# Splitting the first expert's weights during the recurrence instead of during the routing

## The chip, the cores and the metric

One Trainium2 chip, one core. The time is the device time in microseconds of one launch of the whole program; the number that counts is the median of several runs. TensorE is called PE, VectorE DVE, ScalarE ACT, GpSimd POOL, and SyncE, which issues most DMAs, SP.

## The reference

Three layers on N = 10112 tokens (2 sequences of 5056) of width 256. First a gated recurrence, then two mixture-of-experts layers with 8 experts each and one expert per token:

```
f = lower_bound + (1 - lower_bound) * sigmoid(f_logit);  i = 1 - f
h_t = f_t * h_(t-1) + i_t * x_t                      # over the sequence
# MoE (twice; the first with normalized rows and embeddings and a temperature)
e = argmax(logits);  g = softmax(logits)[e]
out = g * (relu(h @ w1[e]) @ w2[e])                  # w1: 256 x 1024, w2: 1024 x 256, fp32
```

## The kernel before

The program has one instruction stream per engine, tied together by semaphores that are written out by hand. Three stages follow one another.

**Recurrence.** The 79 tiles of 128 tokens are taken in 20 chunks (`NCH`) of 4 tiles. For chunk k, PE transposes x and f_logit (`a_front`, L1203), in two halves of 128 features; ACT takes the tanh `th` of the gate half (L1049), POOL turns it into the gate `fg` (L888), DVE makes the product `gx` (L371) and the scan `hT` (L381). A chunk later `a_back` follows: PE transposes `hT` back (L1216) and multiplies it for the router logits (L1222), ACT copies the rows to `h_rows` (L1059) and takes the eight squares and sums `sq` (L1063), which signals `rows_ok`; DVE copies the logits (`keep_logits`, L389), which signals `lg_kept`. PE's next `a_back` waits for `rows_ok` and, ahead of the logits, for `lg_kept`. On SP, step k issues the loads of chunk k + 4 (`load_chunk`, L737; they wait until the transposes of chunk k are done), and then the store of chunk k (`store_chunk`, L745; it waits for `rows_ok`). Each load or store is 512 KB (1.57 MB a chunk). All engines go through steps 0, 1, 2, ... in order; the first steps are unrolled and the rest are in a loop.

**Routing.** DVE finds the largest logit, counts tokens per expert and builds a table of slots with one-hot products on PE (L1240). `slot_row` (L485) tells which row of the scratch tensor `rows_a` goes to which slot. POOL copies two columns of it for each pair of tiles (`places`, L950) and gathers the rows with indirect DMAs (`gather`, L966). PE waits for DVE's mark "table read", and then for the gathered rows (L1290).

**Experts.** 94 steps (47 pairs of tiles per layer), each with the weights of one expert. All products are in fp32r in three parts: a weight matrix is split into a high part, which ACT copies from `w1raw` to `w1h` (`split_w1_hi`, L1032) or from `w2raw` to `w2h` (`split_w2_hi`, L1040), and a low part, the difference, which DVE writes to `w1l` (`split_w1_lo`, L355) or `w2l` (`split_w2_lo`, L362). Each split is two instructions of 128 x 1024. In the steps, the weights of the next expert are loaded and split beside the matmuls of this one (L1306 for the first product, L1324 for the second). For the first pair (`Index(0)`, always expert 0) this has to be done ahead of the steps: SP issues the two loads of 1 MB (L759, L767) behind the store of the last chunk, ACT splits the high parts at the start of its routing, and DVE the low parts between `slot_row` and the mark "table read":

```
link(v.scalar_tensor_tensor(slot_row[:, :], v0, float(P), v1, ALU.mult, ALU.add))
mark["slots"] = count[0]
for c in range(DC):
    split_w1_lo(Index(0), c)
for half in range(2):
    split_w2_lo(Index(0), half)
link(v.tensor_scalar(empty[:, :], v1, 0.0, None, ALU.is_equal))
mark["table read"] = count[0]
```

The constant `SPLIT_K` is 3 and is used nowhere in this kernel but in an assertion.

Of the kernel before, what the change touches and what calls it, by code (L numbers as in the profile page):

```python
# [31 lines left out]
def wait(eng, sem, value):  # L32

    if isinstance(value, int) and value <= 0:
        return
    eng.wait_ge(sem, value)
# [16 lines left out]
def build(nc, x, f_logit, lower_bound, emb, tau, w1a, w2a, w_gate, w1b, w2b, out):  # L53
# [9 lines left out]
    DC = D // P  # L63
# [8 lines left out]
    NCH = -(-TT // CH)  # L72
# [12 lines left out]
    def tiles_in(k):  # L85
        return min(CH, TT - k * CH)
# [10 lines left out]
    with ctx:  # L97
# [178 lines left out]
        def layer_of(i):  # L276
            return loop_layer[0] if i.var is not None else i.const // NP

        def par(i):
            return i.const % 2  # L280

        def pair_uses(i, slots=2, scale=16):
            return i.uses(slots, scale)
# [27 lines left out]
        SPLIT_K = 3  # L311
# [6 lines left out]
        def _(dve):  # L318
            count = [0]

            def link(ins):

                ins.then_inc(dve_c, 1)
                count[0] += 1
                dve.wait_ge(dve_c, count[0])
# [25 lines left out]
            def split_w1_lo(i, c):  # L351

                cols = slice(c * F, (c + 1) * F)
                wait(dve, w1_hi, i.value(2, c + 1))
                v.tensor_tensor(w1l[:, par(i), cols], w1raw[:, par(i), cols],  # L355
                                w1h[:, par(i), cols].bitcast(fp32), ALU.subtract).then_inc(w1_lo, 1)

            def split_w2_lo(i, half):

                cols = slice(half * (WE // 2), (half + 1) * (WE // 2))  # L360
                wait(dve, w2_hi, i.value(2, half + 1))
                v.tensor_tensor(w2l[:, par(i), cols], w2raw[:, par(i), cols],  # L362
                                w2h[:, par(i), cols].bitcast(fp32), ALU.subtract).then_inc(w2_lo, 1)


            def a_step(i, nt=CH, edge=None):
                w = nt * P
                par = i.const % 2
                for c in range(DC):
                    wait(dve, f_ok, i.value(2, c + 1))  # L370
                    v.scalar_tensor_tensor(gx[:, c, 0:w], fg[:, c, 0:w], 1.0, bank[c][:, 0:w],  # L371
                                           ALU.subtract, ALU.mult).then_inc(g_ok, 1)
                    wait(dve, g_ok, i.value(2, c + 1))
                    if edge is not None:

                        link(v.memset(fg[:, c, edge:edge + 1], 0.0))

                    wait(dve, lg_ok, i.value(1, -1))
                    wait(dve, rows_ok, i.value(1, -1))
                    wait(dve, h_ok, i.value(2, c - 1))  # L380
                    v.tensor_tensor_scan(hT[:, c, par, 0:w], fg[:, c, 0:w], gx[:, c, 0:w],  # L381
                                         hT[:, c, 1 - par, CW - 1:CW], ALU.mult,
                                         ALU.subtract).then_inc(h_ok, 1)
                if i.var is not None or i.const > 0:
                    keep_logits(i.plus(-1), CH)

            def keep_logits(k, nt):
                wait(dve, lg_ok, k.value(1, 1))
                v.tensor_copy(logit[:, bass.ds(k.value(CH), nt), :],  # L389
                              bank[6][:, 0:nt * E].rearrange("p (t e) -> p t e", e=E)  # L390
                              ).then_inc(lg_kept, 1)
# [10 lines left out]
            def routing():  # L402
# [81 lines left out]

                link(v.scalar_tensor_tensor(slot_row[:, :], v0, float(P), v1, ALU.mult, ALU.add))  # L485
                mark["slots"] = count[0]
                for c in range(DC):
                    split_w1_lo(Index(0), c)
                for half in range(2):
                    split_w2_lo(Index(0), half)  # L490
                link(v.tensor_scalar(empty[:, :], v1, 0.0, None, ALU.is_equal))
                mark["table read"] = count[0]

# [230 lines left out]
        def _(sp):  # L724
# [6 lines left out]
            def load_chunk(k, nt):  # L731

                slot_x = k.const % XS
                wait(sp, turned, k.value(2, 2 - 2 * XS))
                k0 = k.value(CH)
                for dst, src in ((xin, x_v), (fin, f_v)):
                    sp.dma_start(dst[:, slot_x, 0:nt * D].rearrange("p (t d) -> p t d", d=D),  # L737
                                 src[:, bass.ds(k0, nt), :]).then_inc(xf_in[slot_x], 16)

            def store_chunk(k, nt):  # L740

                par = k.const % 2
                wait(sp, rows_ok, k.value(1, 1))
                k0 = k.value(CH)
                sp.dma_start(rows_av[:, bass.ds(k0, nt), 0:D],  # L745
                             h_rows[:, par, 0:nt * D].rearrange("p (t d) -> p t d", d=D)
                             ).then_inc(h_out[par], 16)
# [3 lines left out]
            def first_expert(i):  # L751
                return i.var is None and i.const == 0

            def load_w1(i):

                w1 = weights[layer_of(i)][0]
                wait(sp, w1_lo, i.value(2, -2))
                src = w1[0:1, :, :] if first_expert(i) else w1[bass.ds(expert_of(i), 1), :, :]
                sp.dma_start(w1raw[:, par(i), :].rearrange("p (c f) -> p c f", c=DC),  # L759
                             src.rearrange("o (c p) f -> p (o c) f", p=P)).then_inc(w1_in[par(i)], 16)  # L760

            def load_w2(i):

                w2 = weights[layer_of(i)][1]
                wait(sp, w2_lo, i.value(2, -2))
                src = w2[0:1, :, :] if first_expert(i) else w2[bass.ds(expert_of(i), 1), :, :]
                sp.dma_start(w2raw[:, par(i), :].rearrange("p (c d) -> p c d", c=FC),  # L767
                             src.rearrange("o (c p) d -> p (o c) d", p=P)).then_inc(w2_in[par(i)], 16)
# [6 lines left out]
            def expert_of(i):  # L775
                return sp.snap(expert_reg[par(i)], min_val=0, max_val=E - 1)
# [9 lines left out]
            def a_step(i):  # L786
                whole = i.var is not None
                if whole or i.const + XS < NCH:
                    load_chunk(i.plus(XS), CH if whole else tiles_in(i.const + XS))
                store_chunk(i, CH if whole else tiles_in(i.const))  # L790
                if i.var is None and i.const == NCH - 1:
                    load_w1(Index(0))
                    load_w2(Index(0))

            run_steps(sp, 0, NCH, a_step, LOOP_K - 3, 5)

            def store_y(i):
# [222 lines left out]
        def _(act):  # L1020
# [6 lines left out]
            def split_w1_hi(i, c):  # L1027

                cols = slice(c * F, (c + 1) * F)
                wait(act, w1_in[par(i)], pair_uses(i) + 16)  # L1030
                wait(act, up_ok, i.value(JS, -JS))
                nc.scalar.activation(w1h[:, par(i), cols], w1raw[:, par(i), cols],  # L1032
                                     ACT.Copy).then_inc(w1_hi, 1)

            def split_w2_hi(i, half):

                cols = slice(half * (WE // 2), (half + 1) * (WE // 2))
                wait(act, w2_in[par(i)], pair_uses(i) + 16)
                wait(act, down_ok, i.value(JS, -JS))
                nc.scalar.activation(w2h[:, par(i), cols], w2raw[:, par(i), cols],  # L1040
                                     ACT.Copy).then_inc(w2_hi, 1)


            def a_front(k, nt):
                w = nt * P
                for c in range(DC):
                    wait(act, turned, k.value(2, c + 1))
                    wait(act, f_ok, k.value(2, c - 1))
                    nc.scalar.activation(th[:, c, 0:w], bank[2 + c][:, 0:w], ACT.Tanh,  # L1049
                                         scale=0.5).then_inc(tanh_ok, 1)  # L1050
# [15 lines left out]

            def a_step(i):
                a_front(i, CH if i.var is not None else tiles_in(i.const))
                if i.var is not None or i.const > 0:
                    a_back(i.plus(-1), CH)  # L1070

# [9 lines left out]

            def routing():

                for c in range(DC):
                    split_w1_hi(Index(0), c)
                for half in range(2):
                    split_w2_hi(Index(0), half)
                act.wait_ge(lg_ok, NCH)
                act.wait_ge(shift_ok, 2)
                nc.scalar.activation(ex[:, 0:TT, :], shifted[:, 0:TT, :], ACT.Exp).then_inc(act_s, 1)  # L1090
                for q, t0 in enumerate(range(0, TT, RC)):
                    scaled(q, min(RC, TT - t0), ST)
# [317 lines left out]
```

## Time and profile before

| | |
|---|---|
| median of 3 runs | 1382.35 us (1382.05 to 1383.36) |
| profiled execution: time / span | 1383.36 / 1381.6 us |
| busy: PE / DVE / ACT / POOL | 96% / 70% / 60% / 32% of the span |
| recurrence | to about 112 us |
| routing | about 112 to 169 us |
| experts | 169 us to the end |
| bytes moved | 276.83 MB, mean 200 GB/s |

A row of the timeline gives start, duration, engine (PEld is the weight load of PE, SPq the issue of a DMA on SP), line, operation, output and inputs, the count of instructions merged into it, and in brackets the idle time of the engine ahead of it with what ended it. Times in it count from the start of the span. "x2 ... 2.36" is two instructions that together took 2.36 us.

### The profile page before, as it was taken

The page shows a single profiled execution, that of the slowest core. Times are in us where ns is not written, and L with a number is a line of the kernel's source. Part 1 is how long each engine was busy: PE and PEld are TensorE (multiplying, and loading weights), DVE is VectorE, ACT ScalarE, POOL GpSimd, SP SyncE. Part 2 cuts the span into 40 slices and gives each one's busy share as a digit, 9 for nine tenths or more (in the row PEclk, how much of TensorE's full clock was granted, in tenths as well). Part 3 has the DMA queues.
Part 4 walks back from the last instruction along what each step waited for, and adds up shares of the span by engine and source line. Part 5 has one row for each costly group of instructions (what it writes and reads, how often), then busy time and mean ns, then how long its engine had stood idle before and what let it go on. Part 6 is the DMA issues. An engine that isn't in the chain of part 4 may idle for free.

```text
span 1381.6 us, 31343 instructions
## 1 busy us (share of the span) xinstructions
PE 1329.6 (96%) x11005; PEld 1299.6 (94%) x11005; DVE 971.5 (70%) x1468; ACT 835.2 (60%) x1402; POOL 439.2 (32%) x458
## 2 busy tenths in 40 slices
PE   7994799999999999999999999999999999999996
PEld 6993399999999999999999999899999999999996
DVE  5878476666666666669876679777777777777773
ACT  4774166666666666666656566556666666666663
POOL 4663221121221211222111234323444444444431
PEclk9995599999999999999999999999999999999999
DMA  8983686666665656668856668546666666666650
GB/s 256 329 275 104 64 273 193 213 199 194 203 198 200 199 195 214 198 193 154 254 166 192 209 202 217 174 153 212 221 217 213 226 226 216 221 213 219 222 186 1
DMA packets 204662, 276.83 MB, mean 200 GB/s; under 512 B 33350, under 2 KB 171988, under 8 KB 204596
## 3 DMA queue, kind: packets, MB, share of 16 engines
q1 hardware_dynamic: 191060, 240.74, 56.7%
q0 software_dynamic: 13536, 35.21, 7.6%
q8 instruction: 41, 0.67, 0.2%
q14 instruction: 25, 0.20, 0.1%
HBM read 242.69 MB, written 35.18 MB: 201 GB/s over the span
## 4 chain that ended last, share of the span: by engine, by line
PE 91%; DVE 4%; issue 1%; ACT 1%; POOL 1%; DMA 1%; SPq 0%; ACTq 0%; DVEq 0%; POOLq 0%
PE bank L1306 39%; PE bank L1324 38%; PE bank L1240 4%; PE bank L1290 3%; PE bank L1335 2%; PE bank L1344 1%; PE bank L1203 1%; PE bank L1222 1%; PE bank L1216 1%; DVE hT L381 1%; DVE gx L371 1%; POOL fg L888 1%; ACT sq L1063 0%; DMA fin<-in_f_logit 0%; ACT th L1049 0%
## 5 line engine op out<-in xcount | busy, mean ns | idle before, releaser
L1306 PE MATMUL bank<-xs,w1h 128*128 128x256 f32 x3008 | 570.5, 288 | 1.5 <-DVE xs L656 1.5
L1119 ACT ACTIVATE hh<-bank 128x512 fp32r<-128x512 f32 x376 | 225.2, 599 | 413.6 <-PE bank L1306 413.6
L1306 PEld LDWEIGHTS bank<-xs,w1h 128*128 128x128 f32 x3008 | 461.5, 189 | 3.2 <-DVE xs L656 1.9
L667 DVE SCALAR_TENSOR_TENSOR hl<-bank,hh 128x512 fp32r<-128x512 f32 x376 | 259.9, 691 | 249.3 <-ACT hh L1119 246.9
L1324 PE MATMUL bank<-w2h,hl 128*128 128x256 f32 x1504 | 423.1, 281 | 0.0
L1324 PE MATMUL bank<-w2l,hh 128*128 128x256 f32 x1504 | 422.5, 281 | 0.0
L1324 PE MATMUL bank<-w2h,hh 128*128 128x256 f32 x1504 | 421.7, 280 | 0.0
L1306 PE MATMUL bank<-xs,w1l 128*128 128x256 f32 x1504 | 421.6, 280 | 0.0
L1306 PEld LDWEIGHTS bank<-xs,w1l 128*128 128x128 f32 x1504 | 283.7, 189 | 0.0
L1324 PEld LDWEIGHTS bank<-w2h,hh 128*128 128x128 f32 x1504 | 283.3, 188 | 0.0
L1324 PEld LDWEIGHTS bank<-w2l,hh 128*128 128x128 f32 x1504 | 283.1, 188 | 0.0
L1324 PEld LDWEIGHTS bank<-w2h,hl 128*128 128x128 f32 x1504 | 283.0, 188 | 0.0
L355 DVE TENSOR_TENSOR w1l<-w1raw,w1h 128x1024 fp32r<-128x1024 f32 x188 | 230.2, 1225 | 45.0 <-ACT w1h L1032 44.8
L362 DVE TENSOR_TENSOR w2l<-w2raw,w2h 128x1024 fp32r<-128x1024 f32 x188 | 230.4, 1226 | 43.1 <-ACT w2h L1040 42.2
L966 POOL DMA_INDIRECT xb<-rows_a,row_i x94 | 110.2, 1172 | 459.1 <-DVE meta L660 440.8
L976 POOL DMA_INDIRECT out_y<-yb,tok x94 | 125.8, 1338 | 313.0 <-DVE tok L675 282.9
L1032 ACT ACTIVATE w1h<-w1raw 128x1024 fp32r<-128x1024 f32 x188 | 197.6, 1052 | 7.1 <-DMA w1raw<-in_moe_w 7.1
L1040 ACT ACTIVATE w2h<-w2raw 128x1024 fp32r<-128x1024 f32 x188 | 197.6, 1052 | 0.8 <-DMA w2raw<-in_moe_w 0.8
L966 POOL DMA_INDIRECT xb<-rows_b,row_i x94 | 107.7, 1146 | 67.0 <-DVE meta L660 29.7
L1135 ACT ACTIVATE yb<-bank,meta 128x256 f32<-128x256 f32 x188 | 78.6, 470 | 11.4 <-PE bank L1324 4.5
L656 DVE TENSOR_TENSOR xs<-bank,xs 128x512 fp32r<-128x512 f32 x94 | 64.9, 690 | 11.5 <-ACT xs L1113 8.9
L1240 PE MATMUL bank<-vals,lane_oh 128*128 128x124 bf16 (+2 forms) x237 | 59.3, 415 | 10.7 <-DVE vals L511 10.5
(160 smaller groups left out, 1039.6 us busy)
## 6 DMA issues: line engine op xcount, KB each, us to landing
w1raw<-in_moe_w SPq DMA_DIRECT2D x94, 1024.0 KB
w2raw<-in_moe_w SPq DMA_DIRECT2D x94, 1024.0 KB, 5.6
rows_b<-yb SPq DMA_DIRECT2D x94, 128.0 KB, 2.3
xin<-in_x SPq DMA_DIRECT2D x19, 512.0 KB, 6.0
fin<-in_f_logit SPq DMA_DIRECT2D x19, 512.0 KB, 7.9
rows_a<-h_rows SPq DMA_DIRECT2D x19, 512.0 KB, 5.6
xb<-rows_a,row_i POOLq DMA_INDIRECT x94, 4.9
xb<-rows_b,row_i POOLq DMA_INDIRECT x94, 4.9
```

The costliest lines, as they stand in the source:

```text
L355: v.tensor_tensor(w1l[:, par(i), cols], w1raw[:, par(i), cols], w1h[:, par(i), cols].bitcast(fp32), ALU.subtract).then_inc(w1_lo, 1)
L362: v.tensor_tensor(w2l[:, par(i), cols], w2raw[:, par(i), cols], w2h[:, par(i), cols].bitcast(fp32), ALU.subtract).then_inc(w2_lo, 1)
L667: v.scalar_tensor_tensor(hl[:, j, :], bank[j % UB][:, :], 0.0, hh[:, j, :].bitcast(fp32), ALU.max, ALU.subtract).then_inc(hid_lo, 1)
L966: pool.indirect_dma_start(xb[:, s, :], None, rows_of(i), bass.IndirectOffsetOnAxis(row_i[:, s:s + 1], 0)).then_inc(x_in[s], 16)
L976: pool.indirect_dma_start(out, bass.IndirectOffsetOnAxis(tok[:, s:s + 1], 0), yb[:, s, :], None, bounds_check=N - 1, oob_is_err=False).the ...
L1032: nc.scalar.activation(w1h[:, par(i), cols], w1raw[:, par(i), cols], ACT.Copy).then_inc(w1_hi, 1)
L1040: nc.scalar.activation(w2h[:, par(i), cols], w2raw[:, par(i), cols], ACT.Copy).then_inc(w2_hi, 1)
L1119: nc.scalar.activation(hh[:, j, :], bank[j % UB][:, :], ACT.Relu).then_inc(hid_hi, 1)
L1135: nc.scalar.activation(yb[:, s, :], bank[Y_BANK + par(i)][:, t * D:(t + 1) * D], ACT.Copy, scale=meta[:, bass.ds(in_layer(i).value(2 * G, ...
L1240: ins = mm(bank[b][:, 0:2 * W], lane_oh[:, g % RS, :, t], vals[:, g % RS, 0:2 * W, t], start=first and t == 0, stop=last and t == w - 1)
L1306: ins = mm(bank[j % UB][:, f * GW:(f + 1) * GW], w[:, p, o:o + P], xs[:, p, a, c * GW:(c + 1) * GW], start=k == 0, stop=k == 3 * DC - 1)
L1324: ins = mm(bank[Y_BANK + p][:, t * D:(t + 1) * D], a[:, j, f * GW + t * P:f * GW + (t + 1) * P], w[:, p, o:o + D], start=(j, t, f, k) == ( ...
```

## The change

The first expert's weights are loaded and split during the recurrence. SP issues the load of w1 in its step 0 and the load of w2 in its step 1, each behind the load and the store of that step. ACT splits the high parts of w1 in its step 3, between `a_front(3)` and `a_back(2)`, and those of w2 in its step 4, between `a_front(4)` and `a_back(3)`. DVE splits the low parts in the same steps, behind the scans and ahead of `keep_logits`. They are taken out of the routing of both engines. The instructions themselves, their number and their data stay the same.

```
--- before.py
+++ after.py
@@ DVE, a_step @@
                     v.tensor_tensor_scan(hT[:, c, par, 0:w], fg[:, c, 0:w], gx[:, c, 0:w],
                                          hT[:, c, 1 - par, CW - 1:CW], ALU.mult,
                                          ALU.subtract).then_inc(h_ok, 1)
+                if i.var is None and i.const == SPLIT_K:
+                    for c in range(DC):
+                        split_w1_lo(Index(0), c)
+                if i.var is None and i.const == SPLIT_K + 1:
+                    for half in range(2):
+                        split_w2_lo(Index(0), half)
                 if i.var is not None or i.const > 0:
                     keep_logits(i.plus(-1), CH)
@@ DVE, routing @@
                 mark["slots"] = count[0]
-                for c in range(DC):
-                    split_w1_lo(Index(0), c)
-                for half in range(2):
-                    split_w2_lo(Index(0), half)
                 link(v.tensor_scalar(empty[:, :], v1, 0.0, None, ALU.is_equal))
@@ SP, a_step @@
                 store_chunk(i, CH if whole else tiles_in(i.const))
-                if i.var is None and i.const == NCH - 1:
+                if i.var is None and i.const == 0:
                     load_w1(Index(0))
+                if i.var is None and i.const == 1:
                     load_w2(Index(0))
@@ ACT, a_step @@
                 a_front(i, CH if i.var is not None else tiles_in(i.const))
+                if i.var is None and i.const == SPLIT_K:
+                    for c in range(DC):
+                        split_w1_hi(Index(0), c)
+                if i.var is None and i.const == SPLIT_K + 1:
+                    for half in range(2):
+                        split_w2_hi(Index(0), half)
                 if i.var is not None or i.const > 0:
                     a_back(i.plus(-1), CH)
@@ ACT, routing @@
-                for c in range(DC):
-                    split_w1_hi(Index(0), c)
-                for half in range(2):
-                    split_w2_hi(Index(0), half)
                 act.wait_ge(lg_ok, NCH)
```

## Rows read from the trace of the kernel before

**Rows 1.** The page: busy time and share of each engine, and the chain by line.

```profile
PE 1329.6 (96%) x11005; PEld 1299.6 (94%) x11005; DVE 971.5 (70%) x1468; ACT 835.2 (60%) x1402; POOL 439.2 (32%) x458
...
PE bank L1306 39%; PE bank L1324 38%; PE bank L1240 4%; PE bank L1290 3%; PE bank L1335 2%; PE bank L1344 1%; PE bank L1203 1%; PE bank L1222 1%; PE bank L1216 1%; DVE hT L381 1%; DVE gx L371 1%; POOL fg L888 1%; ACT sq L1063 0%; DMA fin<-in_f_logit 0%; ACT th L1049 0%
```

**Rows 2.** Busy time by window: start:end, length, each engine's busy time, clock, DMA.

```profile
8.00:20.00 12.00, 10.22 (x48) 9.48 (x48) 6.06 (x7) 3.31 (x6) 5.96 (x4) 1.00 1.04 333
...
34.00:38.00 4.00, 3.88 (x36) 3.64 (x35) 3.44 (x5) 3.04 (x12) 3.01 (x3) 1.00 1.10 303
...
88.00:92.00 4.00, 4.00 (x24) 4.00 (x23) 2.42 (x5) 2.04 (x8) 0.79 (x2) 0.57 1.06 326
```

**Rows 3.** The timeline of the recurrence, steps 2 to 6.

```profile
22.07 0.51 SPq L737 DMA_DIRECT2D xin<-in_x  x1
...
26.84 0.51 SPq L737 DMA_DIRECT2D xin<-in_x  x1
...
28.68 1.09 ACT L1059 ACTIVATE h_rows<-bank 128x512 f32<-128x512 f32 x2 [0.72 <-PE bank L1216]
...
30.98 0.24 ACT L1063 ACTIVATION_READ_ACCUMULATOR sq<-bank 128x1 f32 x1
...
31.30 0.60 ACT L1049 ACTIVATE th<-bank 128x512 f32<-128x512 f32 x1
...
31.93 0.17 DVE L389 COPY logit<-bank 128x32 f32<-128x32 f32 x1
...
32.80 0.69 DVE L371 SCALAR_TENSOR_TENSOR gx<-fg,bank 128x512 f32<-128x512 f32 x1 [0.71 <-POOL fg L888]
...
35.81 0.60 ACT L1049 ACTIVATE th<-bank 128x512 f32<-128x512 f32 x1
...
39.40 0.63 PE L1203 MATMUL bank<-ident,xin 128*128 128x128 f32 x4
```

**Rows 4.** The timeline: the first transposes of chunks 16 and 17.

```profile
87.73 0.83 PE L1203 MATMUL bank<-ident,xin 128*128 128x128 f32 x4
...
93.75 0.64 PE L1203 MATMUL bank<-ident,xin 128*128 128x128 f32 x4
```

**Rows 5.** The loads of L737 issued in 20:24, then those of 24:36.

```profile
DMA to landing us min/median/max: 5.9/6.8/7.7
...
DMA to landing us min/median/max: 5.7/7.0/8.3
```

**Rows 6.** The first expert's loads and high splits in the timeline; landing of L767.

```profile
112.83 0.47 SPq L759 DMA_DIRECT2D w1raw<-in_moe_w  x1
...
119.46 2.00 ACT L1032 ACTIVATE w1h<-w1raw 128x1024 fp32r<-128x1024 f32 x2 [7.09 <-DMA w1raw<-in_moe_w]
...
122.28 2.00 ACT L1040 ACTIVATE w2h<-w2raw 128x1024 fp32r<-128x1024 f32 x2 [0.81 <-DMA w2raw<-in_moe_w]
...
DMA to landing us min/median/max: 8.9/8.9/8.9
```

**Rows 7.** The timeline behind the routing tables.

```profile
158.81 2.36 DVE L355 TENSOR_TENSOR w1l<-w1raw,w1h 128x1024 fp32r<-128x1024 f32 x2
...
159.00 2.21 POOL L950 COPY row_i<-slot_row 128x2 int32<-128x2 int32 x2 [36.81 <-DVE slot_row L485]
...
161.09 2.35 DVE L362 TENSOR_TENSOR w2l<-w2raw,w2h 128x1024 fp32r<-128x1024 f32 x2
...
161.40 2.01 POOL L966 DMA_INDIRECT xb<-rows_a,row_i  x1 [0.18 <-POOL row_i L950]
...
163.71 1.32 POOL L966 DMA_INDIRECT xb<-rows_a,row_i  x1 [0.31 <-issue]
```

**Rows 8.** All copies of L950 and gathers of L966: duration min/median/max in ns.

```profile
L950 POOL COPY row_i<-slot_row x94: 183/202/1187, 159.0 to 1323.3; 128x2 int32 x56, 128x2 int32<-128x2 int32 x38
...
L966 POOL DMA_INDIRECT xb<-rows_a,row_i x94: 942/973/2023, 161.4 to 747.4; - x94
```

**Rows 9.** The chain that ended last: the second gather to its landing.

```profile
163.71 3.11 DMA xb<-rows_a,row_i
```

## The prediction

> **What bounds the kernel now.** I read the page first. TensorE (PE) is busy for 96% of the span and holds nearly all of the chain that ended last, three quarters of it in the two expert products (L1306, L1324) [rows 1]. The change touches none of those matmuls. It can only move the time at which they start, so I asked the trace two questions: what paces the recurrence stage, where work is put in, and what the last step before the first expert matmul waits for, where work is taken out.
>
> The busy time by window answers the first. In 34 to 38 us PE is busy 3.88 of 4.00 us, VectorE (DVE) 3.44, ScalarE (ACT) 3.04, and the DMA share is 1.10 [rows 2]. No engine has room for a long instruction. The timeline shows how they hang together: ACT's first tanh of a chunk starts right behind the eight squares of `a_back` (30.98 + 0.24, then th at 31.30), DVE waits 0.71 us for the gate of that tanh, and the same tanh one chunk on starts at 35.81 [rows 3]. From front(6) at 39.40 to front(16) at 87.73 a chunk takes 48.33 / 10 = 4.83 us [rows 3, 4].
>
> For the second question, in the timeline after the routing tables, behind slot_row, DVE does the four low-part splits from 158.81, 2.36 and 2.35 us for two each, until 163.44. GpSimd (POOL) meanwhile needs 2.21 us for two copies of two columns and 2.01 us for its first gather; the medians of these are 0.202 and 0.973 us each [rows 7, 8]. The copies end at 161.21 and the gather at 163.41, each just as a pair of splits ends. The chain that ended last runs through POOL here: gather at 161.40, second gather issued at 163.71 and landed 3.11 us later, at 166.82, and from there to the first expert matmul [rows 7, 9].
>
> **Part 1, taken out of the routing end.** Four DVE splits (4.6 us) go from between `slots` and `table read`. PE's wait for `table read` isn't what it waits for last; the second gather is. So what counts is how much sooner POOL gets through. With medians: copies from 159.00 to 159.40, gap 0.18, gather to 160.6, gap 0.31, gather to 161.9; from the end of issue to landing it now takes 3.11 − 1.32 = 1.79, so landing at 163.7, that is 3.2 us sooner. Against it, the small DVE operations for `empty` and `experts` now start at 158.8 and fall on POOL's work. The second gather shows the price: 1.32 instead of 0.97 [rows 7, 8]. If each of the four POOL instructions is held by 0.35, 1.4 us are lost, and the gain is 1.8. I take **2.8**, between 1.8 and 3.2, since two of those are very short. The second expert's loads, which wait for `experts`, are issued sooner too, but behind the four POOL instructions, and PE shows no wait for weights on the chain.
>
> The Trainium skill, "SBUF — State Buffer", section "SBUF: two separate sides", says that DVE and GpSimd share one port pair as an exclusive lock, and that a DVE instruction with two SBUF inputs holds it whole against a GpSimd instruction that reads SBUF. The splits have two such inputs, and the trace agrees: POOL's 2.21 and 2.01 us end with them. By the rule only the two-input ones among the small operations could still block, which would put the gain near the upper end.
>
> **Part 2, taken out of the routing start.** ACT's four splits ran from 119.46 to 124.28 while the weights landed [rows 6]. DVE is then busy with the counting that sets the path, and waits for nothing of ACT before the one-hots. This gains 0.
>
> **Part 3, put into the recurrence: ACT.** Step 3 gets `split_w1_hi` twice behind its tanhs and before `a_back(2)`; step 4 gets `split_w2_hi` twice before `a_back(3)`. Two cost 2.00 us [rows 6]. ACT is in order, so `h_rows`, the squares, `rows_ok` (hence SP's store and the next loads), and the next chunk's tanhs wait behind them, and more so if the weights aren't there. W1 is issued where the loads of chunk 5 are now (22.07), W2 about 26.9 [rows 3]. When do they land?
> - Lower bound: the same transfers of before, on an emptier queue: w1 at 112.83, used at 119.46, 6.6 us; w2 8.9 us [rows 6]. That gives w1 at 28.7, w2 at 35.8.
> - Upper bound: W1 (1 MB) replaces the 1 MB of chunk 5, whose second half landed 7.7 us after its issue at 22.6 (22.07 + 0.51), at 30.3. W2 replaces chunk 6's 1 MB, landed 8.3 us after 27.4 (26.84 + 0.51), at 35.7, pushed back by W1: 1.05 MB at the 333 GB/s that the queue gave in 8 to 20 us is 3.1 us [rows 2, 5]. That gives 38.8.
> The queue is full here, so I take **38.0** for W2. ACT's own earliest is about 35, so W1's exact landing no longer matters. Then: splits to 40.0, `a_back(3)` takes 31.22 − 28.68 = 2.54, so the tanh of chunk 5 starts at 42.6 instead of 35.81: **6.8 late** (4.6 with W2 at 35.8, 7.6 at 38.8) [rows 3].
>
> **Part 3, DVE.** The low splits add 2.36 and 2.35 us [rows 7] behind the scans, before `keep_logits`, on which PE's next logits wait. They end near 34.4 instead of 32.1, and the gate product of 32.80 starts about 1.9 late; the second pair repeats it: 3.8 [rows 3, 7]. This runs beside ACT's 6.8 and isn't added; it is the floor. Two small waits in the loop (0.71 of DVE, 0.72 of ACT before h_rows, [rows 3]) close up as everyone is late, so I let 1.0 be recovered: 6.8 − 1.0 = **5.8** (from 3.8, the DVE floor, to 7.6).
>
> **Clock.** PE will stand still for some 2 to 3 us twice (until rows(2), until rows(3)). The trace shows one fall of the granted clock in this stage, 0.57 in 88 to 92 us, where PE had barely paused; that chunk took 93.75 − 87.73 = 6.02, 1.2 over the average [rows 2, 4]. I expect one or two falls, partly inside time that PE waits anyway: **0.6** (0 to 2.4). The skill's "TensorE: Matmul & The Clock Gate", "HAM oscillation — how this bites in real kernels", speaks against the change: idle gaps of PE are paid a second time at half clock. By that each gap would cost a whole 1.2, and the result would be some 2 us worse; the one fall of this trace came without such a gap.
>
> **DMA.** 2.1 MB more at 333 GB/s make the later loads 6.3 us late. Chunk 6's landed at 35.7 for a use at 39.40, slack 3.7 [rows 3, 5]. So they need the stage to be at least 2.6 late, and it is 5.8: no added cost, but a floor of 2.6 under any luckier case.
>
> **Sum.** 5.8 + 0.6 − 2.8 = **+3.6 us**. The profiled execution took 1383.36 for a span of 1381.6, so 1387.0 on its own; it is 1.0 above the median of the three. On the median: 1382.35 + 3.6 = **1386.0**. Bounds: 3.8 + 0 − 3.2 = +0.6, and 7.6 + 2.4 − 1.8 = +8.2. 0.2% is 2.8 us, about what can be told from no change.
>
> **Rivals.**
> - *Same mechanism, smaller.* W2 lands near 35.8 and PE's stalls are partly made good: PE's 3.88 of 4.00 leaves 0.12 in 4 us, over 15 chunks of 4.83 some 2 us. Then 3.8 to 5 − 2.8: about +1.5, 1383.9. For it: W1 alone took only 6.6 us. Against: the full queue. Chance 0.30.
> - *Faster.* The splits are hidden, because each of ACT and DVE waits 0.7 us a chunk and the delay is worked off by the end of the stage; only the routing end counts. It decides from the point where the stage ends under 2.8 late. Full hiding gives −2.8, 1379.6. Against it: PE, at 97%, can't catch up, and the loads alone hold a floor of 2.6. Chance 0.08.
> - *The loads become the bound.* Each later chunk waits for its loads after W1 and W2, with less than 333 GB/s for mixed traffic (303 in 34 to 38, [rows 2]), or the clock falls twice at full price: 8 to 11 − 2.8, +6.5, 1388.9. Chance 0.14.
> - *No effect at either end* (POOL is still held, and the stage absorbs): 0.03.
> The forecast itself holds 0.45.
>
> **Range and chances.** The forecast and the two neighbours: 1381.5 to 1390.5. Slower by over 0.2% takes most of the forecast and all of the third rival: 0.57. Within 0.2%: the rest of the forecast, the first rival, the last, some of the second: 0.36. Faster: 0.07.
>
> **What the profile after would show.** Right: w2h starting near 38 behind an ACT wait for w2raw, the squares of chunk 3 ending near 42.6, PE idle for 2 to 3 us around 34 and 41, the stage's last squares some 5 to 7 us later than now; POOL's two copies under 1 us, the second gather landed within 5.5 us of the first copy's start (159.00 to 166.82, 7.8, now). Wrong: ACT doesn't wait for w2raw (then +1 to +2), the offset of the chunks shrinks steadily towards the end of the stage (hidden), or PE waits for xin or fin (loads bound).

## The result

The changed kernel takes 1391.57 us (median of 4, 1390.43 to 1392.94) against 1382.41 us before: a ratio of 1.0067, 95% interval 1.0055 to 1.0081. It is 9.2 us slower, where +3.6 was predicted. Two later measurements, each beside the kernel before on the same chip, gave 1.0069 (1.0055 to 1.0082) and 1.0071 (1.0057 to 1.0085).

The page after, with the lines that answer to [rows 1] and the granted clock in 40 slices:

```profile
span 1390.7 us, 31342 instructions
...
PE 1333.7 (96%) x11005; PEld 1303.6 (94%) x11005; DVE 971.2 (70%) x1468; ACT 834.7 (60%) x1402; POOL 434.4 (31%) x458
...
PEclk9796589999999999999999999999999999999998
```

The clock's row began 9995599 before; now its second slice, 35 to 70 us, reads 7. PE's busy time has grown by 4.1 us (1333.7 against 1329.6) with the same 11005 matmuls. The timeline of the recurrence, beside [rows 3]:

```profile
26.36 0.66 SPq L769 DMA_DIRECT2D w2raw<-in_moe_w  x1
...
28.57 2.01 ACT L1035 ACTIVATE w1h<-w1raw 128x1024 fp32r<-128x1024 f32 x2 [1.13 <-DMA w1raw<-in_moe_w]
```

```profile
31.37 2.33 DVE L355 TENSOR_TENSOR w1l<-w1raw,w1h 128x1024 fp32r<-128x1024 f32 x2
...
33.15 1.06 PE L1221 MATMUL bank<-ident,hT 128*128 128x128 f32 x8 [1.58 <-ACT sq L1066]
...
37.83 2.00 ACT L1043 ACTIVATE w2h<-w2raw 128x1024 fp32r<-128x1024 f32 x2 [3.86 <-DMA w2raw<-in_moe_w]
...
38.92 2.36 DVE L362 TENSOR_TENSOR w2l<-w2raw,w2h 128x1024 fp32r<-128x1024 f32 x2 [0.62 <-ACT w2h L1043]
...
42.12 1.12 ACT L1052 ACTIVATE th<-bank 128x512 f32<-128x512 f32 x2
...
42.41 1.94 PE L1221 MATMUL bank<-ident,hT 128*128 128x128 f32 x8 [2.59 <-ACT sq L1066]
...
44.14 3.42 PE L1227 MATMUL bank<-en_T,hT 128*128 128x8 f32 x16
...
47.42 1.09 PE L1208 MATMUL bank<-ident,xin 128*128 128x128 f32 x4
```

W1 landed before 28.57 (ACT idle 1.13). W2, issued at 26.36, kept ACT idle for 3.86 us, and its first high split starts at 37.83; the forecast had 38.0. The tanhs of chunk 5 follow at 42.12, against 35.81 in [rows 3], 6.3 late (forecast 6.8). PE stood still for 1.58 and 2.59 us for the rows (L1066), where 2 to 3 us twice were forecast. Up to here the forecast holds. Then the sixteen small matmuls of the logits take 3.42 us at 44.14, where the kernel before needs 1.85:

```profile
42.28 1.85 PE L1222 MATMUL bank<-en_T,hT 128*128 128x8 f32 x16
```

The busy time by window (window, its length, busy time of PE, PEld, DVE, ACT, POOL, granted clock, DMA share, GB/s), to set beside [rows 2]:

```profile
32.00:36.00 4.00, 2.85 (x24) 2.88 (x25) 3.38 (x5) 1.98 (x8) 2.41 (x3) 0.92 1.11 295
36.00:40.00 4.00, 3.82 (x18) 3.42 (x18) 3.35 (x4) 2.17 (x3) 0.09 (x1) 0.50 1.10 350
40.00:44.00 4.00, 1.59 (x8) 1.62 (x9) 1.73 (x4) 3.24 (x12) 1.15 (x2) 0.50 1.10 329
44.00:48.00 4.00, 4.00 (x21) 4.00 (x20) 3.68 (x5) 2.54 (x10) 1.34 (x2) 0.50 1.04 304
48.00:52.00 4.00, 4.00 (x21) 4.00 (x20) 0.78 (x2) 1.19 (x2) 0.77 (x1) 0.50 1.08 292
52.00:56.00 4.00, 4.00 (x37) 3.97 (x36) 3.25 (x4) 3.12 (x11) 2.67 (x2) 0.95 0.53 177
```

The clock is at 0.50, 1.2 of 2.4 GHz, through four windows of 4 us, about 17 us in all by the trace's clock record (35.3 to 52.4), although PE is busy for all of 44 to 52 us. I had looked for one or two falls like the one at 88 us [rows 2, 4], which lasts about 3 us.

The other end, the chain that ended last behind the routing tables, and the two issues beside it in the timeline:

```profile
167.38 0.27 DVE slot_row L491
...
167.86 0.70 POOL row_i L953 x2
...
168.77 1.23 POOL xb L969
...
170.30 5.89 DMA xb<-rows_a,row_i
...
178.41 1.65 PE bank L1311 x6
```

```profile
170.28 0.40 SPq L761 DMA_DIRECT2D w1raw<-in_moe_w  x1
```

POOL is free, as forecast: the two copies take 0.69 us instead of 2.21, and the second gather is issued 2.7 us behind the end of slot_row instead of some 4.9 [rows 7]. But it lands 5.89 us later instead of 3.11 [rows 9]. SP issues the second expert's first load at 170.28, together with it. In the kernel before that load is issued at 165.96, 2.25 us behind the second gather (163.71):

```profile
165.96 0.39 SPq L759 DMA_DIRECT2D w1raw<-in_moe_w  x1
```

From the end of slot_row to the first expert matmul the kernel before takes 169.04 − 158.77 = 10.3 us, the changed one 178.41 − 167.63 = 10.8. The end gained nothing and lost 0.5.

### The profile page after: what moved, and what is told of

Read it like the earlier page. It is cut to its first block, busy times and chain, and to the rows that moved or that the text cites. A ratio compares the mean times of both kernels' runs of the same rounds, so it can differ in the third digit from the quotient of the medians.

```text
span 1390.7 us, 31342 instructions
## 1 busy us (share of the span) xinstructions
PE 1333.7 (96%) x11005; PEld 1303.6 (94%) x11005; DVE 971.2 (70%) x1468; ACT 834.7 (60%) x1402; POOL 434.4 (31%) x458
## 4 chain that ended last, share of the span: by engine, by line
PE 91%; DVE 3%; DMA 2%; issue 1%; ACT 1%; POOL 1%; SPq 0%; DVEq 0%; ACTq 0%; POOLq 0%
PE bank L1311 39%; PE bank L1329 38%; PE bank L1245 4%; PE bank L1295 3%; PE bank L1340 2%; PE bank L1349 1%; PE bank L1208 1%; PE bank L1227 1%; PE bank L1221 1%; DMA w2raw<-in_moe_w 1%; DVE gx L371 1%; DVE hT L381 1%; ACT sq L1066 1%; POOL fg L891 0%; DMA xb<-rows_a,row_i 0%
```

## The experiments

The runs were taken in groups, each on one chip, with runs of the kernel before beside them; a ratio is always to those. It can differ a little from the ratio of the two medians that are given with it. One measure goes through all of them, from the profiled execution of each. "2 to 6" is the time from PE's first back transpose of chunk 2 (L1216) to that of chunk 6, which holds all moved work; "2 to 19" goes to the last chunk; "table to matmul" is from the end of slot_row to the first expert matmul. "Low clock" is the time at 1.2 GHz within 2 to 19, without the fall that ends the stage in every run; each of these columns is of one execution only. "vs before" is the ratio of the run times on one chip, with its 95% interval.

| kernel | vs before | 2 to 6 | 2 to 19 | low clock | table to matmul |
|---|---|---|---|---|---|
| before | 1 | 18.8 | 81.3 | 3 | 10.3 |
| changed | 1.0067 (1.0055, 1.0081) | 29.0 | 90.7 | 17 | 10.8 |
| changed, second time | 1.0069 (1.0055, 1.0082) | 27.7 | 90.2 | 14 | 11.0 |
| changed, third time | 1.0071 (1.0057, 1.0085) | 28.7 | 91.9 | 17 | 11.2 |
| changed, loads held | 1.0042 (1.0028, 1.0055) | 25.6 | 87.0 | 10 | 7.7 |
| changed, PE kept busy | 1.0044 (1.0031, 1.0056) | 24.6 | 87.5 | 3 | 10.8 |
| changed, both | 1.0026 (1.0016, 1.0035) | 25.3 | 88.2 | 3 | 7.6 |
| only the loads moved | 1.0034 (1.0024, 1.0045) | 24.2 | 87.1 | 10 | 10.2 |
| only the loads, 4 row slots | 1.0018 (1.0009, 1.0027) | 21.9 | 85.7 | 10 | 10.4 |
| changed, loads at the start | 1.0050 (1.0037, 1.0063) | 24.0 | 88.1 | 14 | 11.6 |
| loads at the start, low splits in the idle time | 1.0022 (1.0013, 1.0032) | 22.1 | 83.3 | 3 | 11.3 |
| before, low splits in the idle time | 1.0006 (0.9997, 1.0015) | 18.8 | 80.2 | 0 | 11.9 |
| before, low splits in the idle time, loads held | 0.9985 (0.9977, 0.9994) | 18.8 | 81.4 | 3 | 7.6 |
| the last one, second time | 0.9975 (0.9966, 0.9985) | 18.8 | 81.6 | 3 | 7.7 |

**The second expert's loads held back.** SP waits for both gathers of the first pair:

```diff
             sp.wait_ge(dve_c, mark["experts"])
+            for t in range(G):
+                sp.wait_ge(x_in[t], 16)
             read_expert(Index(1))
```

> The changed kernel, but SP issues the second expert's loads only once both gathers of the first pair have landed. Theory A (the gain at the routing end was eaten by these loads, which now run ahead of the second gather): second gather issue to landing falls from 5.9 back to about 3.1 us, the first expert matmul comes 2.5 to 3 us sooner, time about 1388.8. Theory B (the gather is slow for another reason, such as POOL's own issue time): landing stays near 5.9, time 1391.6 or somewhat more. A new wait for the second expert's weights in step 1 would show as PE idle near 187 us and cost up to 3.

Measured: 1388.34 us against 1383.41 (ratio 1.0042), and 10.8 became 7.7 in the last column. The second gather is issued at 165.64 and lands 2.80 us later:

```profile
165.64 2.80 DMA xb<-rows_a,row_i
```

Theory A holds; PE shows no wait for the second expert's weights. Part of the better time may be luck, since this profile also has 7 us less of low clock in the same recurrence; the last column doesn't depend on that.

**The routing end alone.** From the kernel before; DVE's low splits go ahead of its wait for the tables, the rest stays:

```diff
+                for c in range(DC):
+                    split_w1_lo(Index(0), c)
+                for half in range(2):
+                    split_w2_lo(Index(0), half)
                 dve.wait_ge(tab_ok, CHUNK0[1])
...
                 mark["slots"] = count[0]
-                for c in range(DC):
-                    split_w1_lo(Index(0), c)
-                for half in range(2):
-                    split_w2_lo(Index(0), half)
```

> The kernel before, with loads and high splits where they were; only the four low splits of the first expert are moved ahead of the wait for the routing tables, where VectorE idles for 8.8 us. This is the routing-end part of the change alone, with the recurrence untouched. Theory A (loads of the second expert ahead of the gather eat the gain): second gather issued some 2.3 us sooner but landing near 5.9 us later, time within 1 us of before, 1382 to 1383. Theory B (the routing end does gain 2.8 and the change lost that much more in the recurrence): 1379.6.

Measured: 1384.53 against 1383.41, ratio 1.0006, not to be told from no change. The chain that ended last has the second gather:

```profile
159.39 6.96 DMA xb<-rows_a,row_i
```

It takes 6.96 us from issue to landing. Theory A: with the recurrence untouched, taking the splits out of POOL's way gives nothing, because it also lets SP issue the loads (here at 159.37) beside the gather. In the last column it even costs 1.6 us (11.9 against 10.3).

**The loads alone.** From the kernel before, SP's two loads of the first expert move to its steps 0 and 1, as in the change; no split moves:

```diff
-                if i.var is None and i.const == NCH - 1:
+                if i.var is None and i.const == 0:
                     load_w1(Index(0))
+                if i.var is None and i.const == 1:
                     load_w2(Index(0))
```

> The kernel before, with only the two loads of the first expert moved to SP's steps 0 and 1; all splits stay where they were. Theory A (recurrence lost by late splits and PE's clock, not by DMA): the later chunks' loads land some 6 us later than before, by 2 to 3 us too late for chunks 6 to 8; cost 1 to 3 us in the recurrence, nothing at the routing end, time 1383.5 to 1385.5, unless a stall lets the clock fall (then 1387 to 1389). Theory B (the loads by themselves are what costs, through contention): 1388 to 1391 with waits for xin or fin in the trace.

Measured: 1388.71 against 1383.41, ratio 1.0034; 4.7 us by the ratio (5.3 between the medians) for 2 MB that nobody uses yet. The time lies where both theory A with a fall of the clock and theory B had it, and doesn't decide between them. What paces the stage is a wait that neither theory named. The timeline, and the row of the waits:

```profile
26.22 3.90 SPq L737 DMA_DIRECT2D xin<-in_x  x1
...
33.86 1.08 ACT L1060 ACTIVATE h_rows<-bank 128x512 f32<-128x512 f32 x2 [2.86 <-DMA rows_a<-h_rows]
...
36.55 1.06 PE L1217 MATMUL bank<-ident,hT 128*128 128x128 f32 x8 [1.67 <-ACT sq L1064]
...
40.07 1.09 PE L1204 MATMUL bank<-ident,xin 128*128 128x128 f32 x4 [0.77 <-DMA fin<-in_f_logit]
...
41.36 1.09 ACT L1060 ACTIVATE h_rows<-bank 128x512 f32<-128x512 f32 x2 [3.98 <-DMA rows_a<-h_rows]
```

```profile
ACT h_rows L1060 <- DMA rows_a<-h_rows: 8.5, 3, 4.0
```

ACT's copy into `h_rows` waits for earlier stores to land, three times, 8.5 us in total, the longest 4.0. `h_rows` has two slots, and `a_back` waits on `h_out` for the store of two chunks ago; that store now stands in the queue behind 1 MB of weights, and the landing of a store takes up to 9.7 us (at most 6.4 in the kernel before, both in 20 to 45 us). SP's own issue of chunk 6's loads takes 3.90 us instead of the 0.51 of [rows 3], which makes the next store late as well. PE's wait for `fin` in this stretch is only 0.77. Two falls of the clock behind these waits, of about 3 us each (39 to 51 us), are part of the cost too. My step on DMA had counted the loads and left out the store.

**The same with four row slots.** Slots 2 and 3 are put into the half of `w1raw` that is unused in this stage:

```diff
+        def h_slot(n, lo, hi):
+            if n < 2:
+                return h_rows[:, n, lo:hi]
+            spare = w1raw[:, 1, :]
+            return spare[:, (n - 2) * CH * D + lo:(n - 2) * CH * D + hi]
...
-                wait(act, h_out[par], k.uses(2, 16))
+                wait(act, h_out[slot], k.uses(4, 16))
```

> As the run with only the loads moved (4.7 us above before, by a ScalarE wait of 8.5 us for earlier row stores in the trace), but the row buffer h_rows has 4 slots instead of 2, the further two in the half of w1raw that the recurrence doesn't use, so that a late store holds nobody up. Theory A (the moved loads cost through the store behind them, which frees the row buffer): 0 to 2 above before. Theory B (they cost through the later chunks' loads): 3 to 5 above before, with PE waiting for fin.

Measured: 1385.12 against 1382.64, ratio 1.0018, +2.5: between theory A (0 to 2) and theory B (3 to 5). The wait of ACT for the stores is gone from the trace, and about half of the cost with it (0.0034 to 0.0018, in two groups of runs, with intervals that overlap at their ends). What is left in this trace is PE waiting for `fin` (2.2 us) and three short falls of the clock; how the rest divides between them isn't shown.

**TensorE kept busy.** The changed kernel, with transposes that nobody reads ahead of two `a_back`s on PE:

```diff
+            def fill(n):
+                for _ in range(n):
+                    nc.tensor.transpose(bank[7][:, 0:P], ident[:, :], ident[:, :])
...
                 a_front(i, CH if i.var is not None else tiles_in(i.const))
+                if i.var is None and i.const == SPLIT_K + 1:
+                    fill(12)
+                if i.var is None and i.const == SPLIT_K + 2:
+                    fill(36)
```

> The changed kernel, with 12 dummy transposes on TensorE ahead of a_back(3) and 36 ahead of a_back(4), into a bank that nobody reads, so that TensorE isn't idle while it waits for ScalarE; nothing else waits for them. Theory A (of the 9 us lost in the recurrence about 4 are matmuls at 1.2 GHz, since the clock fell for 17 us behind TensorE's idle time): granted clock stays 1.00 from 36 to 52 us, time 1386.5 to 1388.5, more work done in less time. Theory B (the clock is not what costs, the engines' chain is): no gain or a loss of 1 to 3 us from the added instructions, 1391 to 1394.

Measured: 1389.73 against 1383.41, ratio 1.0044 where the change has 1.0067 to 1.0071. In its windows and its timeline:

```profile
32.00:36.00 4.00, 3.78 (x34) 3.50 (x32) 3.39 (x6) 0.89 (x2) 3.05 (x3) 1.00 1.10 332
36.00:40.00 4.00, 3.71 (x35) 3.49 (x33) 3.96 (x5) 3.62 (x9) 0.00 (x0) 1.00 1.10 338
40.00:44.00 4.00, 4.00 (x40) 4.00 (x38) 1.87 (x4) 3.35 (x13) 2.50 (x3) 1.00 1.07 337
44.00:48.00 4.00, 3.69 (x33) 3.38 (x34) 3.29 (x6) 2.71 (x10) 1.81 (x3) 1.00 1.06 319
48.00:52.00 4.00, 3.96 (x37) 3.72 (x36) 2.80 (x4) 3.20 (x12) 2.44 (x3) 1.00 1.10 323
```

```profile
37.44 4.09 PE L1233 MATMUL bank<-ident 128*128 128x128 f32 x36
...
41.37 1.04 PE L1221 MATMUL bank<-ident,hT 128*128 128x128 f32 x8
```

The clock stays at 1.00, with 48 instructions more. Theory A on the mechanism; the time is 1.2 us above its interval, in a group whose kernel before was 1.0 us slower too. The stretch from chunk 2 to 6 is 24.6 us: 5.8 over the kernel before, and 4.4 under the changed one. Part of the 4.4 is not the clock: w2h starts 10.1 us behind the back transpose of chunk 2 here (36.38 against 26.31), and 10.8 in the changed kernel (37.83 against 26.99). The ratios of the runs differ by 0.0023 to 0.0027, which is 3.2 to 3.7 us.

**Both cures.** The two edits above in one kernel.

> The changed kernel with both cures together: dummy transposes while TensorE waits in steps 4 and 5, and the second expert's loads held until the first gathers have landed. If the two losses are separate things and add (each took about 3 us off, of 9), 2.5 to 4 above before. If they overlap (each only shifted the clock's fall), 5 to 7 above.

Measured: 1385.40 against 1382.29 (+3.1), ratio 1.0026 (+3.6; by its interval 2.2 to 4.8). They add, as the first of the two theories has it. In this profile w2h starts as late as in the changed kernel (10.85 us behind the back transpose of chunk 2), the clock doesn't fall in 24 to 100 us, and chunk 2 to 6 takes 25.3: 6.5 over the kernel before, 3.7 under the changed one. What is left of the time is about what had been forecast for the change as a whole.

**The changed kernel again**, on the chips of the second and the third group:

> The changed kernel once more, on the chip of this group, since the size of the loss hangs on how long TensorE's clock stays at 1.2 GHz. Theory: some 7 to 10 us above the kernel before, with 10 to 17 us of low clock in 33 to 53 us. A loss under 5 would say that the first measurement was unlucky in the clock.

> The changed kernel on the chip of this group, to stand beside the two others: 9 us above before, as twice already; how long the low clock lasts will differ.

Measured: 1391.78 against 1382.64, and 1391.75 against 1382.29. In these profiles the clock is low for 10 and 14 us between 34 and 52 us, each time in two stretches, and once more for about 3 us later in the stage; the loss isn't the luck of one run.

**Loads at the program's start.** The changed kernel, with the two loads right behind the first four chunks':

```diff
             for k in range(XS):
                 load_chunk(Index(k), CH)
+            load_w1(Index(0))
+            load_w2(Index(0))
```

> The changed kernel with the first expert's loads issued right behind the first four chunks' loads at the program's start, where the DMA queue runs empty at 20 us. Splits as in the change. Theory A (most of the loss in the recurrence is waiting for W2, the row store behind the weights, and the clock that falls with it): ScalarE doesn't wait for w2raw or for the row store; only the splits' own 4 us are left, total 3 to 5.5 above before. Theory B (the splits themselves upset the chain): 7 to 10 above before, as the change.

Measured: 1388.67 against 1382.64, +6.0 between the medians, and +6.9 by the ratio of 1.0050 (5.1 to 8.7 by its interval). That lies between theory A (3 to 5.5) and theory B (7 to 10) and decides for neither. ACT doesn't wait for weights here, and for a store only 0.2 us. Yet the clock still falls, four times for about 3 us. Ahead of the first two falls (35 to 39 and 42 to 46 us) the timeline has only small stalls, PE's logits waiting for `keep_logits`, which stands behind DVE's low splits:

```profile
31.01 2.33 DVE L355 TENSOR_TENSOR w1l<-w1raw,w1h 128x1024 fp32r<-128x1024 f32 x2
...
33.50 2.00 PE L1225 MATMUL bank<-en_T,hT 128*128 128x8 f32 x16 [0.65 <-DVE logit L395]
...
37.84 2.33 DVE L362 TENSOR_TENSOR w2l<-w2raw,w2h 128x1024 fp32r<-128x1024 f32 x2
...
40.34 2.00 PE L1225 MATMUL bank<-en_T,hT 128*128 128x8 f32 x16 [0.55 <-DVE logit L395]
```

That these stalls cause the falls isn't shown: the other two falls, and the one of the kernel before, come without them.

**The same without DVE's part.** The low splits go ahead of the wait for the tables, as in the second experiment; ACT's high splits stay in the recurrence.

> Loads at the program's start and the high splits in the recurrence, as in the run with early loads (6.0 us above before); but the low splits are taken out of the recurrence and stand ahead of the wait for the routing tables. Theory A (VectorE's 4.7 us behind the scans, with the logits that wait for them, pace the rest of the loss; ScalarE's 4 us run beside them): most of the 6 goes, 1 to 3 above before. Theory B (ScalarE's splits pace it, in front of a_back): 4 to 6 above before.

Measured: 1385.22 against 1382.29, ratio 1.0022, +2.9. Theory A: without DVE's splits about half of the loss is gone, the falls of the clock that went with them included (14 us of low clock became 3). From chunk 2 to 6 this kernel costs 22.1 − 18.8 = 3.3 us, for ACT's splits, 1.3 us of its waits for stores, and one short fall of the clock.

**The low splits moved and the loads held.** From the kernel before: low splits in DVE's idle time, and the second expert's loads held until the gathers have landed.

> The kernel before with the low splits ahead of the wait for the routing tables, and SP issuing the second expert's loads only once the first pair's gathers have landed. Theory A (the routing end holds 2 to 3 us that the loads took back): 2 to 3 us under before, second gather landed about 3 us after its issue. Theory B (nothing to gain there, since the first two steps then wait for the second expert's weights): as before within 1 us, with PE idle ahead of step 1.

> The version that came out 2.7 us under the kernel before, once more on another chip or at another time: 2 to 3 us under before if the gain is real, within 1 us if it was drawn from the spread of the runs.

Measured: 1379.94 against 1382.64, ratio 0.9985 (0.9977 to 0.9994), and again 1380.00 against 1384.07, ratio 0.9975 (0.9966 to 0.9985). It is faster than the kernel before both times, by 0.15% and 0.25%. The second gain, 3.5 us by the ratio and 4.1 between the medians, is larger than the 2 to 3 expected, and larger than the 2.6 us that the profile's last column accounts for; why stays open. The timeline of the first of the two has the splits inside an idle stretch that ran to 158 us, the chain has the second gather:

```profile
149.30 2.35 DVE L355 TENSOR_TENSOR w1l<-w1raw,w1h 128x1024 fp32r<-128x1024 f32 x2
...
151.57 2.36 DVE L362 TENSOR_TENSOR w2l<-w2raw,w2h 128x1024 fp32r<-128x1024 f32 x2
```

```profile
161.46 2.69 DMA xb<-rows_a,row_i
...
166.36 4.62 PE bank L1308 x24
```

2.69 us from issue to landing, and 7.6 us from slot_row to the first matmul: 2.7 less than before, nearly the 2.8 that had been forecast for the change. PE shows no wait for the second expert's weights; ACT waits 1.5 us for w2, which holds nobody up.

## Why the prediction was wrong

**Right: what the splits and the late weights do to the chain.** W2 landed at 37.8 (forecast 38.0), the tanh of chunk 5 came 6.3 late (6.8), and with the clock kept up the stage is 5.8 and 6.5 us longer from chunk 2 to 6 in two profiles, for a term of 5.8 in the sum; that one of them gives the same figure is luck. PE's two halts came where they were expected. The routing start gave nothing, as said: from the last back transpose to the end of slot_row it is 49.9 us in both kernels.

**Wrong: the size of the clock's term.** The step that failed: "I expect one or two falls, partly inside time that PE waits anyway: 0.6 (0 to 2.4)". One long stretch of about 17 us at 1.2 GHz followed the halts, and cost some 4 us: 29.0 − 24.6 = 4.4 against the first profile with PE kept busy, 29.0 − 25.3 = 3.7 against the second, whose W2 came as late. How much a low clock costs depends on where it falls. With the loads held, in the same recurrence, the clock was low for 10 us too, and chunk 2 to 6 took 25.6, hardly more than with the clock kept up; in the changed kernel's second profile 10 us went with 27.7. The one fall in the trace of before was taken as the price of any fall. It had come without a halt of PE; behind halts of 1.6 to 2.6 us the clock was low for 10, 14 and 17 us between 34 and 53 us in the three profiles of the change. In the longest of these stretches ACT waited 2.55 us for PE's transposes, and POOL and DVE for ACT in turn, so that PE's matmuls set the pace at half speed. The Trainium skill, "TensorE: Matmul & The Clock Gate", "HAM oscillation — how this bites in real kernels", has idle gaps of PE paid a second time in a slow clock. Its example is a loop that waits longer for its data than it computes, which PE doesn't do here; but it pointed the right way, and its weight was set too low: I had put it at some 2 us worse. In the other direction, the short fall at 88 us [rows 2, 4] is missing in the changed kernel, and gave 1.3 back there: the offset of the back transposes is 10.2 us from chunk 7 to 14 and 8.9 from chunk 15 on. Such short falls come and go from run to run in the same code.

**Wrong: the routing end.** The step that failed is "The second expert's loads ... are issued sooner too, but behind the four POOL instructions". POOL's part was right (2.3 us of the 3.2 at most were gained at the issue), but the loads were issued at 170.28 beside the second gather at 170.30, and its landing took 5.89 instead of 3.11. The forecast gain of 2.8 became a loss of 0.5. Holding the loads gives it back, by 3.1 us in the changed kernel and 4.3 in the other (11.9 to 7.6). In the kernel before, the low splits had kept the loads behind the gathers, by 2.25 us, with nobody having planned it.

**The sum, again.** In the profiled executions, with the split between chain and clock taken from the first profile with PE kept busy: −0.6 from the very start (clock and loads of the first chunks), +5.8 chain, +4.4 clock, +0.6 where chunk 6 to 7 took longer, −1.3 for the fall at 88 us, +0.5 routing end, together +9.4, and the first expert matmul comes 178.41 − 169.04 = 9.4 us later. The forecast was 5.8 + 0.6 − 2.8. The −1.3 is the luck of one execution, not a gain of the change.

**Incomplete: the DMA step.** It gave the moved loads no cost. Alone they cost 4.7 us, about half of it through the store behind them and the two slots of `h_rows`. In the changed kernel ACT shows no wait for the stores; it waits for W2 and does the splits in that time. The rival "the loads become the bound" was the nearest in time (+6.5), but not in its mechanism: PE waited for a load once, 1.4 us, at the program's start (1.1 before). None of the rivals had the gather behind the loads.

**Open.** How much of the 3 to 4 us that both cures leave is ACT's part, and how much DVE's, is known only with early loads (2.9 us with ACT's splits alone). Why the short falls of the clock occur in some executions and not in others, and why the low clock behind the halts lasted 10 us once and 17 another time, wasn't settled.

## What to carry to other kernels

Before moving work into a stage, look at what its engines' halts do to TensorE's clock: in a stage where TensorE is 97% busy, some 6 us of delay cost about 4 more in the changed kernel. When an instruction is taken out of a path, list everything that it held back, transfers on other queues too; here the bulk loads that it had kept behind a latency-bound gather took back the whole gain, and a wait on SP for the gathers recovers it. The place for a few microseconds of off-path work is an engine's own idle stretch that the timeline shows (8.8 us of DVE here), not a stage where PE, DVE and ACT are busy for three quarters of the time or more and the DMA queues are full (34 to 38 us in [rows 2]).

## What the runs showed of the hardware

- The second gather from POOL's queue landed 2.7 to 3.2 us after its issue in the seven profiles in which SP issued its loads of 1 MB 2.2 us or more behind it, and 5.9 to 7.0 us in the seven in which SP issued them at the same time.
- The issue of a 512 KB load on SP, 0.51 us in [rows 3], took 3.90 us where it stood behind both loads of weights (3.60 in the changed kernel), and so held up what SP had to do next.
- The granted clock stayed at 1.2 GHz through 44 to 52 us with TensorE busy in every window (4.00 of 4.00 us) with transposes and 8-column matmuls, while with 48 transposes of nobody's data in PE's waits it stayed at 2.4 GHz there, in both profiles that have them.
- POOL's copies and gathers ended with DVE's two-input splits before (2.21 and 2.01 us) and took 0.69 and 1.23 without them. The Trainium skill, "SBUF — State Buffer", "SBUF: two separate sides", says that such an instruction holds the shared port pair for its whole length; the trace agrees.
